# Scores of a second mixture of experts computed as extra columns of the first one's output product, on one Trainium2 core

## The reference

```python
w  = softmax(weight_gen, axis=-1)                      # 7 taps for each of 8 heads
x0 = sum_k w[:, k] * x[s - 6 + k]                      # a gliding sum per head
# first mixture: noisy gates, two of 8 experts
noisy = x0 @ w_gate + log1p(exp(x0 @ w_noise)) * noise
top2, gates = two largest of noisy, softmax of the two
x1 = sum over the two: gate * (relu(x0 @ w1[e]) @ w2[e])        # w1 192x1024, w2 1024x192
# second mixture: cosine scores against 8 embeddings, one of 8 experts
xn = x1 / (norm(x1) + 1e-6);  en = emb / (norm(emb) + 1e-6)
logits = xn @ en.T / tau
e = argmax(logits);  gate = softmax(logits)[e]
out = gate * (relu(x1 @ v1[e]) @ v2[e])
```

## Time and profile before

| | us |
|---|---|
| median of 3 runs (1159.77 to 1162.67) | 1160.85 |
| the profiled execution | 1162.41 |
| its span | 1160.6 |
| PE busy | 1066.6 (92%) |
| PE weight loads | 1001.3 (86%) |
| DVE busy | 736.6 (63%) |
| POOL busy | 591.5 (51%) |
| ACT busy | 528.1 (46%) |

### The profile page before, as it was taken

How to read it: one execution, slowest core, us unless ns; L and a number is a source line. 1 busy time by engine, 2 the same in 40 slices (tenths; PEclk the granted TensorE clock), 3 DMA queues, 4 the chain that set the end, 5 groups by cost and what they waited for, 6 DMA issues and landing times.

```text
span 1160.6 us, 27731 instructions
## 1 busy us (share of the span) xinstructions
PE 1066.6 (92%) x7861; PEld 1001.3 (86%) x7861; DVE 736.6 (63%) x1504; ACT 528.1 (46%) x1398; POOL 591.5 (51%) x723
## 2 busy tenths in 40 slices
PE   1989469999999999999999999989499999999997
PEld 0566249999999999999999999955299999999997
DVE  8999886565565655656556565547756565567663
ACT  2122465454454544545445454425345454456553
POOL 6888114555565555555555555520134444444443
PEclk9999779999999999999999999989699999999999
DMA  9656874225242442423435335261331331133611
GB/s 327 187 160 169 157 9 99 41 41 105 40 102 41 78 68 38 105 41 70 76 41 104 43 54 92 38 156 53 15 98 39 103 101 41 41 100 97 166 37 31
DMA packets 105846, 98.76 MB, mean 85 GB/s; under 512 B 30899, under 2 KB 96746, under 8 KB 105532
## 3 DMA queue, kind: packets, MB, share of 16 engines
q1 hardware_dynamic: 76412, 62.08, 22.9%
q0 software_dynamic: 29376, 35.97, 18.1%
HBM read 63.82 MB, written 34.98 MB: 85 GB/s over the span
## 4 chain that ended last, share of the span: by engine, by line
PE 84%; DVE 7%; POOL 2%; DMA 2%; issue 2%; ACT 2%; DVEq 0%; POOLq 0%; ACTq 0%; SPq 0%
PE banks L718 23%; PE banks L720 11%; PE banks L704 9%; PE banks L710 7%; PE banks L706 7%; PE banks L709 7%; PE banks L705 7%; PE banks L641 3%; DVE prods L1002 2%; PE banks L687 2%; POOL prods L478 2%; PE banks L622 2%; PE banks L688 2%; ACT hi_rows L931 1%; PE banks L604 1%
## 5 line engine op out<-in xcount | busy, mean ns | idle before, releaser
L1209 DVE SCALAR_TENSOR_TENSOR h_lo<-banks,h_hi 128x256 fp32r<-128x256 f32 x736 | 312.4, 425 | 336.8 <-ACT h_hi L912 332.9
L912 ACT ACTIVATE h_hi<-banks 128x256 fp32r<-128x256 f32 x736 | 282.1, 383 | 422.4 <-PE banks L710 422.3
L718 PE MATMUL banks<-w_hl,h_hi 128*128 128x384 f32 x1472 | 467.0, 354 | 0.0
L720 PE MATMUL banks<-w_hl,h_lo 128*128 128x192 f32 x1472 | 367.9, 250 | 0.0
L720 PEld LDWEIGHTS banks<-w_hl,h_lo 128*128 128x128 f32 x1472 | 280.1, 190 | 0.0
L718 PEld LDWEIGHTS banks<-w_hl,h_hi 128*128 128x128 f32 x1472 | 277.0, 188 | 0.2
L490 POOL DMA_INDIRECT x_slots<-token_rows,gather_idx x188 | 188.7, 1004 | 111.7 <-POOL gather_idx L483 81.2
L509 POOL DMA_INDIRECT token_rows<-y_slots,store_idx x120 | 193.7, 1614 | 84.8 <-POOL store_idx L504 51.7
L704 PE MATMUL banks<-x_hi_a,w_hi 128*128 (+1 forms) x736 | 226.0, 307 | 1.7 <-DVE x_hl_b L1169 1.7
L710 PE MATMUL banks<-x_hl_b,w_lo 128*128 (+1 forms) x736 | 207.5, 282 | 0.0
L709 PE MATMUL banks<-x_hl_b,w_hi 128*128 (+1 forms) x736 | 207.5, 282 | 0.0
(11 more groups left out here) (181 smaller groups left out, 1165.8 us busy)
## 6 DMA issues: line engine op xcount, KB each, us to landing
raw<-in_moe_w SPq DMA_DIRECT2D x17, 768.0 KB
token_rows<-stage SPq DMA_DIRECT2D x28, 384.0 KB, 4.6
raw<-in_moe_w SPq DMA_DIRECT2D x17, 512.0 KB
raw<-in_moe_w SPq DMA_DIRECT2D x34, 256.0 KB
token_rows<-zeros SPq DMA_DIRECT2D x14, 386.0 KB, 6.0
x_halo<-in_x SPq DMA_DIRECT2D x2, 2688.0 KB, 15.6
rows<-token_rows SPq DMA_DIRECT2D x14, 384.0 KB, 7.0
x_slots<-token_rows,gather_idx POOLq DMA_INDIRECT x188
```

The source lines that it names most:

```text
L718: mm(y[:, i, 0:2 * D], h_hi[:, c % HBUFS, t], w2_hl[u][:, c, :, :], start=c == 0, stop=False)
L720: ins = mm(y[:, i, 0:D], h_lo[:, c % HBUFS, t], w2_hl[u][:, c, 0, :], start=False, stop=c == FC - 1)
L912: sc.activation(h_hi[:, c % HBUFS, :], banks[:, c % HBANKS, 0:BLOCK], ACT.Relu).then_inc(h_hi_ready[m], 1)
L1209: v.scalar_tensor_tensor(h_lo[:, c % HBUFS, :], banks[:, c % HBANKS, 0:BLOCK], 0.0, h_hi[:, c % HBUFS, :].bitcast(F32), ALU.max, ALU.subtr ...
```

## The change

The scores of the second mixture are x1 times the scaled embeddings, and x1 is a sum of h @ w2. So the change multiplies each w2[e] with the embeddings once, on chip, and lets the eight resulting columns ride behind w2's 192:

- The host passes `moe_w2` once more, turned (`w2t`). SP loads it as eight transfers of 128 x 1536 floats into `wide`, seven of them while the last attention groups run. PE makes `fold(e)` for each expert: 12 products of 16 columns, four experts before `positions(0)` and four inside it. ACT copies the result into `score_w` and into expert 0's w2; POOL makes expert 0's low part. For the other experts SP copies `score_w[:, e]` into columns 192 to 199 of `raw2`, and the splits of w2 take it along.
- `second_product` in mixture 0 has 400 and 200 columns instead of 384 and 192; y, its buffers and `token_rows[1]` have 200 columns, the last eight of which add up to the scores.
- After mixture 0, SP reads the scores of all tokens with one transfer of 8 floats each and then the rows. The transposes, the score products and their copies are gone. The squared norms are made by ACT, one Square with accumulation per tile: 48 tiles before `hot_rows(1)`, 8 after it. DVE picks over all tokens at once.
- The gate is made after `positions(1)`; its last part comes behind the first split of mixture 1. SP stores the gates in a table of their own, `gate_rows`, and POOL gathers them for each block with two indirect transfers of 128 x 1 float.

```diff
@@ SP
+                if g == NG - 1:
+                    sp.wait_ge(second_prods, NG)
+                    for e in range(E - 1):
+                        sp.dma_start(wide[:, e, :], w2t[e]).then_inc(fold_in[e], 16)
...
+            sp.dma_start(wide[:, E - 1, :], w2t[E - 1]).then_inc(fold_in[E - 1], 16)
+            sp.wait_ge(gates_ready[0], 1)
+            for k in range(CHOICES[0]):
+                sp.dma_start(tile_rows(token_rows[0], k * T, T)[:, :, D:D + 1], gate[k][:].unsqueeze(2),
...
             with sp.Fori(2, E) as e:
                 sp.wait_ge(weights_ready, e)
                 load_expert(w1, w2, e)
+                load_score_weights(e)
...
+            sp.dma_start(logits[:, :, 0:E], tile_rows(token_rows[1], 0, T)[:, :, D:DS]).then_inc(scores_in, 16)
             for g in range(NG):
                 sp.dma_start(rows[:, g * GROUP:(g + 1) * GROUP, :], tile_rows(token_rows[1], g * GROUP, GROUP)[:, :, 0:D]).then_inc(x1_in[g], 16)
             sp.wait_ge(gates_ready[1], 1)
-            store_gates(1)
+            for b in range(B):
+                sp.dma_start(gate_rows[b * S:(b + 1) * S].rearrange("(p j) o -> p (j o)", p=P), gate[0][:, b * J:(b + 1) * J]).then_inc(gates_stored[1], 16)
@@ GpSimd, mixture
+                def gather_gates(n):
+
+                    gp.tensor_copy(gate_idx[:], gate_at[:, bass.ds(n * HALVES, HALVES)]).then_inc(gate_idx_copied, 1)
+                    pool.wait_ge(gate_idx_copied, n + 1)
+                    pool.sem_inc(pool_tick, 1)
+                    for i in range(HALVES):
+                        gp.indirect_dma_start(gate_in[:, i:i + 1], None, gate_rows,
+                                              bass.IndirectOffsetOnAxis(gate_idx[:, i:i + 1], 0)).then_inc(gates_landed, 16)
+                def take_landed_gates(n):
+
+                    at = n % RING * HALVES
+                    pool.wait_ge(gates_landed, n * 32 + 32)
+                    pool.sem_inc(pool_tick, 1)
+                    gp.tensor_copy(gate_ring[:, bass.ds(at if isinstance(n, int) else pool.snap(at), HALVES)], gate_in[:]).then_inc(gates_taken[1], 1)
+                    pool.wait_ge(gates_taken[1], n + 1)
+                    pool.sem_inc(pool_tick, 1)
                 def gather_before(g):
                     pool.wait_ge(x_turned[m], g + 3)
                     pool.sem_inc(pool_tick, 1)
-                    take_gates(g + 2)
+                    if m == 0:
+                        take_gates(g + 2)
                     gather(g + 3)
...
                     gather_start()
+                    if m == 1:
+                        take_landed_gates(g + 1)
+                        gather_gates(g + 2)
...
+                if m == 1:
+                    pool.wait_ge(ids_ready[1], 2)
+                    pool.wait_ge(gates_stored[1], 16 * B)
+                    gather_gates(0)
+                    take_landed_gates(0)
+                    gather_gates(1)
                 full = pool.snap(pool.value_load(full_blocks[m][0:1, :], min_val=E - 3, max_val=MAXB[m] - 3))
@@ TensorE
+            def fold(e):
+
+                pe.wait_ge(fold_in[e], 16)
+                for c in range(FC // 2):
+                    for r in range(THIRDS):
+                        at = (r * FC // 2 + c) * P
+                        ins = mm(banks[:, 6, (e * FC + 2 * c) * E:(e * FC + 2 * c + 2) * E], wide[:, e, at:at + P], emb_t3[:, r, :],
+                                 start=r == 0, stop=r == THIRDS - 1)
+                ins.then_inc(folded, 1)
...
-                        mm(y[:, i, 0:2 * D], h_hi[:, c % HBUFS, t], w2_hl[u][:, c, :, :],
+                        mm(y[:, i, 0:2 * WIDTH[m]], h_hi[:, c % HBUFS, t], w2_hl[u][:, c, :, 0:WIDTH[m]],
                            start=c == 0, stop=False)
-                        ins = mm(y[:, i, 0:D], h_lo[:, c % HBUFS, t], w2_hl[u][:, c, 0, :],
+                        ins = mm(y[:, i, 0:WIDTH[m]], h_lo[:, c % HBUFS, t], w2_hl[u][:, c, 0, 0:WIDTH[m]],
                                  start=False, stop=c == FC - 1)
...
             mixture(0)
-            pe.wait_ge(emb_ready, 1)
-            keep_clock(26)
-            for g in range(NG):
-                turn_rows(1, g, g % 2, rows[:, g * GROUP:(g + 1) * GROUP])
-                if g > 0:
-                    group_scores(g - 1)
-                if g > 1:
-                    turn_scores(g - 2)
...
             positions(1)
@@ ScalarE
+            act.wait_ge(folded, E)
+            product = banks[:, 6, :].rearrange("p (e c o) -> p e c o", c=FC, o=E)
+            sc.copy(score_w[:], product).then_inc(score_w_ready, 1)
+            sc.copy(w2_hl[0][:, :, 0, D:DS], product[:, 0]).then_inc(first_score_hi, 1)
             hot_rows(0)
             mixture(0)
...
+            def norms(groups):
+                for g in groups:
+                    act.wait_ge(x1_in[g], 16)
+                    for t in range(g * GROUP, (g + 1) * GROUP):
+                        sc.activation(rows[:, t, :], rows[:, t, :], ACT.Square, accum_out=sumsq[:, t:t + 1]).then_inc(norm_made, 1)
+
+            norms(range(NORMS_FIRST))
+            hot_rows(1)
+            norms(range(NORMS_FIRST, NG))
+            act.wait_ge(norm_made, T)
             sc.sqrt(inv_norm[:], sumsq[:]).then_inc(roots_ready, 1)
+            sc.activation(table_probe[:], quad_scale[:, 0:1], ACT.Exp)
             act.wait_ge(route_ask[1], 1)
             sc.activation(r["noisy"][:], r["noisy"][:], ACT.Exp).then_inc(route_act[1], 1)
-            hot_rows(1)
             mixture(1)
@@ VectorE
+            dve.wait_ge(scores_in, 16)
+            pick(0, scores)
...
-            positions(1, weigh_best, finish_best)
-            mixture(1)
+            positions(1)
+            weigh_best()
+            mixture(1, finish_best)
```

More of the change, by code:

```diff
@@ L30 @@
 EMB_AT = 6
+EMB_TURN_AT = 8
+FOLD_FIRST = 4
+NORMS_FIRST = 12
 EARLY_GROUPS = 11
@@ L152, in attention_moe_moe @@
         gate_sum = sb("gate_sum", [P, T])
+        r.update({n: sb(n, [P, T, E]) for n in ("soft_d",)})
+        r.update(soft_u=r["tie"], soft_w=r["pos"], soft_ln=r["picked"])
+        wide = sb("wide", [P, E, FOLD])
+        rows = wide[:].rearrange("p e c -> p (e c)")[:, 0:T * D].rearrange("p (t d) -> p t d", d=D)
+        member = sb("member", [P, T, E], BF16)
+        counts = sb("counts", [P, E, T])
+        cum = sb("cum", [P, 1 + E * T])
         totals = sb("totals", [P, E])
@@ L230, in attention_moe_moe @@
         rows_ready = sem("rows_ready")
[L231 to L234, removed]
+        rows_turned = sem("rows_turned")
+        rows_t_ready = sem("rows_t_ready")
+        logits_done = sem("logits_done")
+        logits_ready = sem("logits_ready")
         rows_stored = [sem(f"rows_stored{u}") for u in range(2)]
@@ L670, in positions @@
                 mm(banks[:, 1, 0:T * E], ones[:], flat, start=True, stop=True).then_inc(ranks_done[m], 1)
+                if m == 0:
+                    for e in range(FOLD_FIRST, E):
+                        fold(e)
                 cols = HI_COLS[m]
@@ L885, in split_next @@
                     else:
-                        f = slice(2 * (c - half), 2 * (c - half) + 2)
-                        sc.copy(w2_hl[1 - u][:, f, 0, :], raw2[:, f, :]).then_inc(weight_hi, 1)
+                        scored = m == 0 and expert < E - 1
+                        if scored and c == half:
+                            act.wait_ge(score_cols_in, 16 * (expert + 1))
+                        f, width = slice(2 * (c - half), 2 * (c - half) + 2), DS if scored else D
+                        sc.copy(w2_hl[1 - u][:, f, 0, 0:width], raw2[:, f, 0:width]).then_inc(weight_hi, 1)
                 def take_half(g, i, last=False):
@@ L1186, in split_next @@
                         f = slice(2 * (c - half), 2 * (c - half) + 2)
-                        ins = v.tensor_tensor(w2_hl[1 - u][:, f, 1, :], raw2[:, f, :], w2_hl[1 - u][:, f, 0, :].bitcast(F32), ALU.subtract)
+                        width = DS if m == 0 and expert < E - 1 else D
+                        ins = v.tensor_tensor(w2_hl[1 - u][:, f, 1, 0:width], raw2[:, f, 0:width], w2_hl[1 - u][:, f, 0, 0:width].bitcast(F32), ALU.subtract)
                         if c == FC - 1:
@@ L1230, in _ @@
             positions(0, weigh_pairs, finish_pairs)
-            v.memset(y_slots[:, :, :, D:D + 1], 0.0).then_inc(pads_zeroed, 1)
             mixture(0)
-            for g in range(NG):
-                dve.wait_ge(x1_in[g], 16)
-                if g > 0:
-                    dve.wait_ge(norms_ready, g)
-                tiles = slice(g * GROUP, (g + 1) * GROUP)
-                step(v.tensor_tensor(square[:], rows[:, tiles, :], rows[:, tiles, :], ALU.mult))
-                v.tensor_reduce(sumsq[:, tiles], square[:], AX.X, ALU.add).then_inc(norms_ready, 1)
-            scores = logits[:, :, 0:E]
-            for first, last in ((0, EARLY_GROUPS), (EARLY_GROUPS, NG)):
-                dve.wait_ge(logits_ready[1], last)
```

(8 more changed lines are left out.)

246 lines of the change are left out of this document (115 added, 131 removed).

## The result

The changed kernel takes 1208.74 us (median of 5 runs, 1204.51 to 1210.4), the kernel before 1160.99 beside it: the ratio is 1.0393, with a 95% interval of 1.038 to 1.0407. The forecast was 1177.0 with a range of 1151 to 1190. The direction was right, the size was not: +47.8 us instead of +16. The profiled execution is the fastest of the five (1204.51, span 1202.5), so the traces account for 42 of the 48 us; the rest is scatter between executions (the first one-hot rows start at 168.0 in this trace, at 169.3 to 169.4 in those of runs 2, 3 and 5, which have the same code up to there).

What follows compares the result with a forecast made beforehand. The prediction took TensorE, 92% busy, to bound the kernel, with GpSimd becoming the second mixture's bound after the change. Terms +2.5, +6.4, -19.2 and +26.7 gave +16.4 us on 1160.85: 1177 us, range 1151 to 1190.

Steps and rivals of the forecast that it cites:

- Part 1, the folding: Ahead of the first mixture: folding embeddings into w2 delays the first one-hot rows, +2.5 us (0 to 5).
- the last transfer's landing: In the folding: the eighth transfer lands near 146.5, then one fold and ScalarE's copies precede the one-hot rows.
- Part 2: First mixture: wider second products cost +6.4 us (5 to 9.6); the long product pays 16 columns, the short one's 8 are free.
- Part 3: Between the mixtures: reading back, transposes, score products and pick leave TensorE, -19.2 us (-30 to -12).
- scores and first rows: Between the mixtures: scores land 9 us after the first mixture's last row lands, the first row group 1.3 us later.
- squares 0.46: Between the mixtures: ScalarE's Square and accumulator read take 0.46 us a tile, 22.1 us for 48 tiles before the one-hot rows.
- the tail 1.7: Behind the second routing's one-hot rows: ScalarE's remaining work delays block 0 by 0 to 4 us, taken as 1.7.
- a sign of being wrong: The forecast would be wrong if squares pipeline with their accumulator reads, or 4 B gathers issue in half a microsecond.
- ScalarE being out of the way: Between the mixtures: ScalarE's norms do not hold the one-hot rows, gain 30; as a rival 1166 us, chance 0.11.
- Part 4: Second mixture: gate gathers lengthen GpSimd's iteration to 10.7 us against TensorE's 9.78, making GpSimd the bound, +26.7 us (0 to 35).
- The late start of 2.6: Second mixture's start: GpSimd's iteration 0 begins at 855.0 instead of 852.42 because of the first gate gathers, +2.6 us.
- The end, forecast at -2.7: Second mixture's end: GpSimd's slack is given back once, -2.7 us.

Runs made afterwards that it cites:

- run 2: Changed kernel, but from block 3 of the second mixture gates come with the rows, as a column of the row table: 1167.38 us.
- run 3: Changed kernel, but VectorE leaves out the low parts of the experts' weights in the second mixture: 1198.65 us.
- run 5: Changed kernel, but the first mixture's short product (h_lo) has 192 columns again instead of 200: 1209.72 us.
- run 9: Changed kernel with its fold as it was, plus one dense 512-column product behind every six fold passes, 32 in all: 1212.88 us.
- run 4: Changed kernel with the fold's operands exchanged: embeddings loaded as weights, 3 products of 512 columns an expert instead of 12, result turned by transposes: 1189.81 us.
- run 1: Changed kernel, but the second mixture gathers only the first half's gates per block and scales both halves with them: 1167.32 us.
- run 7: run 6 plus gates in a row-table column, stored behind block 3's rows, with gates of blocks 0 to 3 still gathered separately: 1151.89 us, ratio 0.9916.
- run 6: run 4 with the eighth fold and its copies moved behind the first routing's one-hot rows, and TensorE's warm-up cut from 22 products to 8: 1186.17 us.
- run 10: run 7, but gates of blocks 0 to 5 are gathered separately and the column is stored only behind block 5's rows: 1166.3 us.

## Why the prediction was wrong

**Part 1, the folding, is the step that failed.** It said "One fold has 12 loads and products; 12 such loads took 1.42 us". The count of 12 is that of the products in the source, but the 12 entries of the earlier trace rows are only six float32 products; a fold has 24 entries. And the price came from passes between dense products, at a clock of 1.00; these ran at 0.50. Eight folds took 19.5 + 20.5 = 40.0 us, not 8 x 1.42 = 11.4. At the price of run 9's passes before the clock fell (0.67 / 6 = 0.11), 192 passes would be about 21 us, an estimate; so the count and the clock each nearly double the price. With it the path was wrong: the forecast let the last transfer's landing hold the one-hot rows, with only the last fold behind it, and said nothing of the ranks, which the first four folds held. The term had 2.5, its bounds ended at 5, and it cost 20.8; run 4 took 15.9 of it back in the traces (18.9 in the medians) with the same transfers. (The term's own sum was also loose: 146.5 + 1.4 + 0.8 is 148.7, not 148.9.)

**Part 2** was right: +6.2 for +6.4, with run 5 for the short product. TensorE's weight loads in the first mixture, after, start 0.18 and 0.11 us apart, where the earlier trace rows had 0.17 and 0.11; over the whole mixture the medians are 0.183 instead of 0.176 while a long product runs, and 0.110 as before while a short one runs:

```profile
253.06 0.19 PEld L775 LDWEIGHTS banks<-w_hl,h_lo 128*128 128x128 f32 x1
253.24 0.19 PEld L773 LDWEIGHTS banks<-w_hl,h_hi 128*128 128x128 f32 x1
253.35 0.19 PEld L775 LDWEIGHTS banks<-w_hl,h_lo 128*128 128x128 f32 x1
```

**Part 3** had the right order and mechanism (ScalarE later than VectorE, by 5 us instead of 10.7) and was mis-sized in its terms: scores and first rows 3.2 us too late, squares 0.46 for 0.35 a tile (5.3 us), the tail 1.7 for 0.9. That squares pipeline with their accumulator reads was named as a sign of being wrong, and they do. The gain was 28.7, near the bound of 30 that was given for ScalarE being out of the way, and yet ScalarE was in the way.

**Part 4** had the right mechanism and the right ordinary iteration; GpSimd did become the bound (runs 1 and 2). The term was mis-sized by 17: the mean period 11.03 instead of 10.7 gives 29 x 0.33 = 9.6. VectorE's weight work is the larger part (run 3: 7.9 by the traces, 10.1 by the medians); the wait for landing gates in iteration 0 and the idle time in the iteration of 12.6 add 2.5 and 2.1, and the ordinary iteration, a little shorter than 10.7, takes some back. The late start of 2.6 was in fact nothing: iteration 0 came 14.0 us behind the first product, as before. The end, forecast at -2.7, was +7.8: 1202.5 - 1170.01 = 32.5 against 24.7 in the earlier trace rows. The slack was not given back: GpSimd waited 2.49 us for gates once more, and 5.4 of the 7.8 lie behind the last store (below), where the forecast had nothing.

Parts 1 and 4 together cost 36 us more than forecast; part 3 gave 9.5 more back, which was luck for the total.

Run 7 says what the idea itself is worth: with the fold turned and no gathers of gates in the iteration, the same score columns make the kernel 0.8% faster than before. It also has the shorter warm-up of run 6, which the kernel before lacks; but its first product comes at 174.7, not 173.6, so that is not where the gain lies.

## What to carry to other kernels

Count float32 products in the trace, not in the source, and take their price from a stretch in which TensorE does the same kind of work, with its clock read beside it. When an engine's serial iteration passes the bound, its mean counts, with everything that lengthens single iterations; removing one small transfer from it may be worth thirty times its own duration, since the loop pays it every time (1.27 us and 38 in run 1). Before a transfer of thousands of small pieces is put between gathers, look for who waits for those gathers.

## What the runs showed of the hardware

- TensorE, busy without a gap, can sit at the low clock: 16-column float32 passes went at 0.50 (0.203 us each), 512-column ones in the same place at 1.00 (0.44 us each).
- VectorE's subtraction with both inputs in SBUF lengthened GpSimd's indirect transfers by 0.3 us each (0.97 to 1.29, 1.01 to 1.31; run 3 removes it).
- At the 356th indirect transfer GpSimd starts late for no reason that the profile shows, in the kernel before (2.27 us idle), the changed one (2.15) and runs 1, 3 and 5 (3.51, 2.15 and 2.15), whatever that transfer is. Its cause stays open.
- From the end of GpSimd's last store to the end of the span 3.1 us pass in the kernel before, 8.6 in the changed one and in run 3, 5.9 with one gate gather a block (run 1), 2.5 in run 7, 10.9 in run 10. GpSimd's closing drain, which is no part of its busy time, is what differs: 1.55 us before, 6.94 in the changed kernel, 4.32 in run 1, 0.89 in run 7, 9.22 in run 10. It does not follow the number of indirect transfers that a kernel has issued (372, 436, 404, 380 and 384). Its cause stays open; no run was made for it. The changed kernel's last store:

```profile
1192.95 0.98 POOL L561 DMA_INDIRECT out_rows<-y_slots,store_idx  x1 [0.30 <-issue]
```
